# Attention on one core: the transposes of the probabilities in another word type

## The reference, cut to what matters

```python
mask = q_bucket[:, :, :, None] == k_bucket[:, :, None, :]
scores = scale * np.matmul(q, k.transpose(0, 1, 3, 2))
scores = np.where(mask, scores, -1000000000.0)
scores = scores - np.max(scores, axis=-1, keepdims=True)
attn = np.exp(scores)
attn = attn / (np.sum(attn, axis=-1, keepdims=True) + 1e-09)
return np.matmul(attn, v).astype(np.float32)
```

## Time and profile before

| what | value |
|---|---|
| median of 3 runs | 643.7 us (640.82, 643.7, 644.79) |
| the profiled execution, time | 640.22 us |
| the profiled execution, span of its instructions | 638.2 us |
| granted TensorE clock, mean | 0.998 |
| attention stage | up to about 252 us of the span |

### The profile page before, as it was taken

One profiled execution on the slowest core, in us unless ns is written; L12 is line 12 of the kernel. 1 busy time (PEld: TensorE's weight loads), 2 busy tenths in 40 slices (PEclk: granted clock), 3 DMA queues, 4 the chain that ended last, 5 costly groups with the idle time before them and its releaser, 6 DMA issues.

```text
span 638.2 us, 11468 instructions
## 1 busy us (share of the span) xinstructions
PE 618.2 (97%) x4384; PEld 483.7 (76%) x4384; DVE 361.1 (57%) x1132; ACT 295.3 (46%) x525; POOL 146.9 (23%) x152
## 2 busy tenths in 40 slices
PE   7899999999999999888999999999999899999996
PEld 3777777777777776367998989998999877777773
DVE  6877677767776676887868778786512220000000
ACT  5777777777777776542525344352212111111111
POOL 5340303030312921210110101010333124333201
PEclk9999999999999999999999999999999999999999
DMA  8938936365454200271634435373799869999970
GB/s 180 235 78 177 221 81 156 90 146 120 113 180 103 50 13 1 100 275 64 240 132 158 158 132 183 131 255 111 259 330 324 283 210 330 355 349 350 324 275 20
DMA packets 73393, 116.38 MB, mean 182 GB/s; under 512 B 33799, under 2 KB 37161, under 8 KB 73058
## 3 DMA queue, kind: packets, MB, share of 16 engines
q1 hardware_dynamic: 68738, 106.75, 54.7%
q0 software_dynamic: 4016, 8.80, 4.0%
q10 hardware_dynamic: 576, 0.01, 0.0%
HBM read 87.76 MB, written 12.23 MB: 157 GB/s over the span
## 4 chain that ended last, share of the span: by engine, by line
PE 87%; DMA 5%; DVE 3%; SPq 2%; issue 2%; ACT 1%; POOL 0%; POOLq 0%; DVEq 0%
PE psB L1064 13%; PE psB L1078 11%; PE psB L353 10%; PE psB L338 9%; PE psB L1810 9%; PE psB L1825 9%; PE psA L323 6%; PE psA L325 5%; PE psB L368 2%; DMA q_in<-in_q 2%; PE psA L1000 2%; DMA x_scratch<-x 1%; PE psB L281 1%; DMA xg<-x_scratch,recs 1%; PE psB L1101 1%
## 5 line engine op out<-in xcount | busy, mean ns | idle before, releaser
L474 DVE TENSOR_REDUCE mx<-psA 128x1 f32<-128x768 f32 x96 | 91.9, 957 | 52.2 <-PE psA L325 50.5
L542 ACT ACTIVATE prob<-psA,ebi,esc 128x768 f32<-128x768 f32 x96 | 95.3, 993 | 24.1 <-DVE ebi L419 19.8
L1064 PE MATMUL psB<-xgT,w 128*128 128x192 f32 x512 | 91.9, 332 | 0.3 <-ACT xgT L1164 0.3
L1078 PE MATMUL psB<-hT,w 128*128 128x192 f32 x512 | 88.2, 329 | 0.0
L1064 PEld LDWEIGHTS psB<-xgT,w 128*128 128x128 f32 x512 | 82.5, 190 | 7.4 <-issue 3.6
L1078 PEld LDWEIGHTS psB<-hT,w 128*128 128x128 f32 x512 | 82.7, 190 | 0.3
L338 PE MATMUL psB<-cst,prob 128*128 128x128 f32 x576 | 78.7, 273 | 0.2
L323 PE MATMUL psA<-kH,qT 128*128 128x384 f32 x192 | 74.2, 386 | 3.3 <-ACT kB L581 1.6
L338 PEld LDWEIGHTS psB<-cst,prob 128*128 128x128 f32 x576 | 66.9, 140 | 5.0 <-DVE pT L487 1.5
L353 PE MATMUL psB<-pT,v_in 128*64 128x384 f32 x360 | 68.0, 499 | 0.0
L593 ACT COPY pT<-psB 128x512 f32<-128x512 f32 x96 | 56.0, 583 | 25.4 <-PE psB L338 24.6
(11 more groups left out here) (289 smaller groups left out, 840.1 us busy)
## 6 DMA issues: line engine op xcount, KB each, us to landing
w<-in_moe_w SPq DMA_DIRECT2D x34, 2048.0 KB, 10.4
kH<-hi SPq DMA_DIRECT2D x30, 192.0 KB
q_in<-in_q SPq DMA_DIRECT2D x16, 192.0 KB, 4.0
k_in<-in_k SPq DMA_DIRECT2D x16, 192.0 KB, 4.2
v_in<-in_v SPq DMA_DIRECT2D x8, 384.0 KB, 3.6
x_scratch<-x_of_batch SPq DMA_DIRECT2D x2, 1536.0 KB, 6.7
x_scratch<-x SPq DMA_DIRECT2D x8, 384.0 KB, 10.4
qT<-hi SPq DMA_DIRECT2D x15, 192.0 KB
```

What stands on the lines that cost most here:

```text
L474: nc.vector.tensor_reduce(mx[:, u:u + 1], psS[u % 2][:, :, 0:HALF], AX.XY, ALU.max).then_inc(s_dv, 1)
L542: nc.scalar.activation(prob[:, u % 2, :, :], psS[u % 2][:, :, 0:HALF], ACT.Exp, bias=ebi[:, u:u + 1], scale=esc[:, u:u + 1], accum_out=den ...
L1064: ins = nc.tensor.matmul(ps[:, (f % 2) * CAP:(f % 2 + 1) * CAP], w1[:, k % 2, d, f * P:(f + 1) * P], xgT[:, k % 2, d, :], start=d == 0, st ...
L1078: ins = nc.tensor.matmul(ps[:, (d % 2) * CAP:(d % 2 + 1) * CAP], w2[:, k % 2, f, d * P:(d + 1) * P], hT[:, k % 2, f, :], start=f == 0, sto ...
```

## The change

The words, the identity and the result of the transposes in step T are named float32r. The exponentials are still written as float32: the name `prob` is kept for a float32 tensor that is released at once, and `prob_words` is float32r in the same place. The result in the bank is float32r by a cast of the name alone; its readers read float32. The identity needs a copy that is written as float32r; GpSimd makes it ahead of the memsets, after a wait for the constants, and counts it in `s_ze`, for whose 5 TensorE and SP now wait.

```diff
-    prob = sb("prob", [P, 2, 2, HALF], F32)
+    with nc.sbuf_tensor("prob", [P, 2, 2, HALF], F32) as prob:
+        pass
+    probR = sb("prob_words", [P, 2, 2, HALF], F32R)
+    idR = sb("identity_words", [P, P], F32R)
...
         if pair == 1:
-            sp.wait_ge(s_ze, 4)
+            sp.wait_ge(s_ze, 5)
...
                 if u == 0:
-                    pe.wait_ge(s_ze, 4)
+                    pe.wait_ge(s_ze, 5)
...
-                        ins = nc.tensor.transpose(psT[part][:, at * P:(at + 1) * P],
-                                                  prob[:, u % 2, c // GU, c % GU * P:(c % GU + 1) * P],
-                                                  cst[:, C_ID:C_ID + P])
+                        ins = nc.tensor.transpose(psT[part][:, at * P:(at + 1) * P].bitcast(F32R),
+                                                  probR[:, u % 2, c // GU, c % GU * P:(c % GU + 1) * P],
+                                                  idR[:, :])
...
+        gp.wait_ge(K["s_const"], 16)
+        nc.gpsimd.tensor_copy(idR[:, :], cst[:, C_ID:C_ID + P]).then_inc(s_ze, 1)
+        gp.wait_ge(s_ze, 1)
         for n, t in enumerate((qB[96:128, 0], kB[96:128, 0], qB[64:128, 1], kB[64:128, 1])):
             nc.gpsimd.memset(t.bitcast(F32), 0.0).then_inc(s_ze, 1)
-            gp.wait_ge(s_ze, n + 1)
+            gp.wait_ge(s_ze, n + 2)
```

## The result

The changed kernel takes 633.4 us (median of 4 runs, 631.5 to 636.8) against 642.8 us for the kernel before in the same comparison: a ratio of 0.9861, 95% interval 0.9829 to 0.9893. Timed again on another chip it is 631.6 against 640.5 us, 0.9860 (0.9832 to 0.9887). So the gain is some 9 us, 1.4% (9.4 us between the medians of the first comparison, 8.9 in the second). Its profiled execution took 632.04 us, with a span of 630.0, where the one before had 640.22 and 638.2.

The account below looks back on a forecast made before the run. TensorE was taken to bound the attention stage, so shorter transpose slots save kernel time. 11.5 us saved less 0.5 at the start gave 629.2 us profiled, 632.5 as median (likeliest case 0.38); range 618 to 647.

Parts of the forecast that it names:

- The slot: Attention-stage transposes on TensorE: one starts every 0.084 us instead of 0.110, the middle of two ends, saving 0.026 us each.
- The lower end: Transpose slot at one moving column per cycle, as in the float32r score products: 0.058 us for 128 columns.
- What of it counts: Five distances in each of 96 units save 12.5 us; with those before V, 13.7, of which 11.5 remain after 2.2 given back.
- Before V: Distance from a transpose to the products with V: 45 of them shrink by 0.026 us each, 1.2 us together.
- nothing changes before a score product: Distance from a unit's last transpose to a following score product: set by that product's own load, 0.11 us, so nothing saved.
- What is late next: Gaps between units without products with V: VectorE's copy lets at most 0.17 us go; they shrink by 0.13, so cover holds.
- The sign that I had named: In the changed profile, the row of transposes' waits for VectorE's copy grows only if the slot is at its lower end.
- The start: GpSimd's identity copy and wait for constants delay memsets, q's first split and placement DMAs: 0.5 us, bounds 0 and 1.4.
- The sum: Whole kernel: profiled 640.2 - 11.5 + 0.5 = 629.2 us; against the 643.7 median 632.7, stated as 632.5.
- Full: Rival: transposes' moving side and load both at one column per cycle, slot 0.058 us, kernel 621 to 625 us; chance 0.22.
- no change: Rival: the 0.112 us load or two halves of a word keep the transpose slot; 643 to 646 us; chance 0.31.
- slower: Rival: transposes run as ordinary two-record products, 0.224 us each, 66 us more, about 705 us; chance 0.09.

Follow-up runs that it names:

- 0.060 alone: Separate kernel computing nothing of the reference, issuing runs of 24 transposes or products of one form: 0.060 us per float32r slot with 64 or 32 columns loaded, 128 moving.
- The 72 slots of prep: Changed kernel with the identity's copy behind the memsets and the 72 q and k transposes for pairs 2 to 7 also float32r: 630.95 us, 0.9856 of the kernel before.
- The copy alone: Changed kernel with its transposes back in float32, leaving only the identity's copy and its wait ahead of the memsets: 640.95 us, 1.0008 of the kernel before.
- 1.2 us won in the expert stage: Changed kernel with late identity copy, 72 q and k transposes and 128 first-expert-stage transposes also float32r: 632.85 us, 0.9883 of the kernel before.
- the swapped banks: Changed kernel with ScalarE's four transposes of a unit first and VectorE's two last: 629.75 us, 0.9837 of the kernel before.
- the repeat: The changed kernel as it is, run again beside the start variants: 631.6 us, 0.9860 of the kernel before.

## Why the prediction was right, point by point

- **The slot.** Predicted 0.084 us, between 0.058 and 0.110; measured 0.0846 as the mean of all 480 distances (0.1095 before). The size was right, its reason was not derived: I took the middle of two ends, and that the load fell there is luck. The lower end's moving side was right (0.060 alone and after a score product). But the load follows neither row that I had: 0.085 us for 128 words, not 0.06 as from the bf16 loads, nor 0.112 as from the float32r ones outside of transposes. Of the two rules of the Trainium skill ("TensorE: Matmul & The Clock Gate"), the fourfold rate of the section Terms would be a slot of 0.056 us, which no row of 128-column transposes in 32-bit words reached. The load rule of the section LDWEIGHTS, 107 ns for 128 columns, fails in transposes at 0.063 (float32) and 0.085 us (float32r); outside of them, 0.111 us for the plain float32r product is near it. It was right in one thing: after this change the load decides.
- **What of it counts.** 12.5 us for the distances inside the units: measured 480 x (0.1095 - 0.0846) = 12.0. Before V 0.026 us each: measured 0.025 (8.5 to 7.5 us over 42). That nothing changes before a score product was wrong. Its load now starts some 0.05 us after the last transpose's start (124.43 to 124.48) instead of with it, and this distance grew by 1.8 us in sum, of which the 1.6 us less after a prep take back most.
- **What is late next.** Here lies the term that was mis-sized. I gave each gap without V 0.17 us of cover and let all of them shrink by 0.13. Their medians went from 1.38 to 1.32 and from 1.37 to 1.37 us, and the 24 of them in units 12 to 95 gave 0.05 us in sum (33.79 to 33.74), where 24 x 0.13 = 3.1 was forecast; one of them, at 176 us, grew by 0.38, in its wait for ScalarE. I had read the cover at one gap (0.22 us from the copy's end to the transposes); the other kind has 0.13, and both need 0.05 of it for the semaphore. So the working gave too much for one kind, and for the first as well: there the maximum, and with it the copy, starts later against the transposes ahead of it once these are quicker (0.83 instead of 0.75 us from their start to the copy's). VectorE's maximum, its copy and the semaphore bound the gap from then on. The waits come back partly in the long gaps, which shrank more (3.32 to 3.05 and 3.12); an undisturbed pair gained 1.48 instead of the forecast 1.72 us, and the whole of units 12 to 95 gained 8.9, where the same working gives 11.5. The 72 slots of prep, taken off as well, made it no shorter. The sign that I had named, the row of waits growing only at the lower end of the slot, was wrong too: it grew from 1.5 to 5.1 us at a slot in the middle.
- **The start.** 0.5 us predicted, with 0 as a bound. The copy alone shows 1.0008, 0.5 us, with 0.2% to either side, so the comparisons can't tell 0.5 from 0; in its trace nothing of the delay is left at unit 12. GpSimd's shift was as worked out (memsets until 8.68 us, first split at 8.74), but the first scores were late by VectorE's cast, which the prediction didn't have, and the delay was absorbed in the wait for DMA.
- **The sum.** 11.0 us predicted; 8.2 between the profiled executions and 8.9 to 9.4 between the medians. The gain is so 1.6 to 2.1 us smaller than forecast, and the time is nearer to it (633.4 against 632.5) only because the kernel before measured 642.8 in the comparison and not the 643.7 from which I had started; that part is luck. From the first instruction to unit 95 the profile has 9.7 us less (248.94 to 239.26): 8.9 in units 12 to 95, and 0.8 ahead of them, where I had counted 0.5 more and no saving. From there to the end it has 1.5 us more (389.3 and 390.8), in work that the change doesn't touch. This part lies between 388.6 and 391.3 us in the executions of all kernels here, at 390.8 and 388.6 in the two of the changed one itself, so I take that for scatter. In six of them, with and without the change, some 1.7 us of it is a stretch at half clock between 271 and 288 us.
- **The rivals.** Full and no change are ruled out by the slot; slower, a transpose in two records, by their number: 576, as before. (Its time was added up from the profiled execution; from the median its 66 us give some 709 us, not 705.)

## What to carry to other kernels

In these runs a slot on TensorE is the larger of the moving side and the load, each with its own price by type, so halving one brings only what the other leaves: time both, by varying one count of columns at a time, before a type is changed. TensorE busy in all of a window doesn't prove that it is the bound: read what every step starts after, at each kind of gap, and take the smallest cover. When a change brings less than its arithmetic, look for the waits that were covered before, and for the granted clock behind the place that got shorter; here moving one wait made the next one show, and 1.2 us won in the expert stage went to a slower clock right behind it.

## What the runs showed of the hardware that I had not expected

- Naming the words float32r halves the moving side of a transpose (0.109 to 0.060 us for 128 columns) but makes its load slower: 0.085 us for 128 columns where float32 takes 0.062 (with 64 or 32 rows). The profile's own duration of a load is 140 ns for both and doesn't show it; only the distances do.
- VectorE's casts from SBUF to SBUF and GpSimd's instructions shut each other out, and which one pays is decided by which starts first. A cast of VectorE that starts inside a memset or a two-input operation of GpSimd ends 0.41 to 0.42 us after it, in 16 cases of 16 in the first 16 us of the kept traces (0.62 to 1.59 us instead of 0.55; five are behind the memset, in all five traces that have the copy ahead). The other way round, GpSimd's cast of q, where it starts inside VectorE's cast or while this one is held up, ends 0.68 to 0.69 us after it, in 12 cases of 12: 1.18 us in the kernel before, where a cast of the same shape alone takes 0.83. There VectorE's had started 0.05 us ahead and kept its 0.55:

```profile
7.41 0.55 DVE L455 CAST qT<-raw 64x768 fp32r<-64x768 f32 x1
```

  VectorE's copies out of `psA` beside the same memsets take 0.55 to 0.56 us, no more than elsewhere. The Trainium skill ("GPSIMD Engine Reference", section 1. Specifications, the row on SBUF interfaces) states that GpSimd shares its interfaces with VectorE, with contention for an instruction in a two-port mode or with two inputs from SBUF; these traces agree for the memset, the two-input operation and the cast, if the casts ran in such a mode, which the trace doesn't show.
- In three of the five kept traces with the copy ahead of the memsets, TensorE's granted clock falls below full speed for a stretch of the start; in the other two, the copy alone and the swapped banks, it doesn't, so the late first scores don't bring it by themselves. Windows of the changed kernel:

```profile
0.00:14.00 14.00, 9.82 (x38) 4.90 (x39) 7.77 (x15) 6.06 (x9) 9.59 (x12) 0.88 0.76 171
14.00:20.00 6.00, 5.58 (x37) 4.19 (x35) 5.53 (x13) 3.98 (x8) 1.99 (x3) 1.00 1.09 266
```

  Six transposes of k that took 0.87 us take 1.49 there, at the lower of the two levels. In that execution TensorE had waited 1.25 us for q before its first transposes, 0.56 before the change. In the repeat the first of these windows has 1.00 and the second 0.72. None of the traces with early first scores has such a stretch at the start. What brings it about is not shown.
